# A Fourier mixer and feed-forward kernel: unrolled, with 502-token tiles and a transposed output product

## The reference

```python
X = np.fft.rfft(x, axis=1)                       # along the 3008 tokens
Yr = Xr @ w_r - Xi @ w_i + b_r                   # 256 x 256 weights
Yi = Xr @ w_i + Xi @ w_r + b_i
Y = sign(Y) * maximum(abs(Y) - 0.01, 0)          # of each part
y = np.fft.irfft(Y, n=3008, axis=1)
h = y @ w_in                                     # 256 -> 2048
g = np.maximum(h, 0) + alpha * np.minimum(h, 0)  # alpha: one per hidden unit
out = g @ w_out                                  # 2048 -> 256
```

## Time and profile before

| | |
|---|---|
| median of 3 runs | 1544.65 us (1544.44 to 1545.94) |
| profiled execution, span from first to last instruction | 1542.4 us |
| TensorE matmuls | busy 1452.6 us (94%), 10262 |
| VectorE | 1009.4 us (65%), 2117 |
| ScalarE | 770.3 us (50%), 1901 |
| GpSimd | 232.6 us (15%), 193 |
| DMA | 83.47 MB in 64545 packets, mean 54 GB/s |
| granted TensorE clock, mean | 0.976 |

### The profile page before, as it was taken

The page is one execution under the profiler, slowest core; times in us unless marked ns, Lnnn a source line. Parts: engine busy times, 40 slices in busy tenths (PEclk is TensorE's granted clock), DMA queues, the critical chain, the costliest instruction groups (busy, mean ns, idle before and its releaser), DMA issues.

```text
span 1542.4 us, 33926 instructions
## 1 busy us (share of the span) xinstructions
PE 1452.6 (94%) x10262; PEld 1421.0 (92%) x10262; DVE 1009.4 (65%) x2117; ACT 770.3 (50%) x1901; POOL 232.6 (15%) x193
## 2 busy tenths in 40 slices
PE   2368979999999999999999999999999999999998
PEld 1157879999999999999999999999999999999998
DVE  2247767777677677777677777677767655565654
ACT  1134445555555555555555555555554554555443
POOL 0034431111111111111111111111101010000000
PEclk9997779999999999999999999999999999999999
DMA  2345541111111111111111011111010000000000
GB/s 81 106 143 160 169 130 52 62 48 58 56 50 42 49 61 61 61 48 59 56 50 35 27 41 41 41 41 41 30 41 30 32 21 27 25 20 20 20 10 21
DMA packets 64545, 83.47 MB, mean 54 GB/s; under 512 B 6912, under 2 KB 48256, under 8 KB 64512
## 3 DMA queue, kind: packets, MB, share of 16 engines
q1 hardware_dynamic: 62384, 79.49, 16.5%
q10 hardware_dynamic: 2128, 3.58, 0.7%
...
## 4 chain that ended last, share of the span: by engine, by line
PE 85%; issue 0%; ACT 0%; ACTq 0%
PE out_ps L337 35%; PE h_ps L337 35%; PE work_ps L337 9%; PE work_ps L423 2%; PE work_ps L375 1%; PE work_ps L425 1%; PE work_ps L377 1%; ACT ffw_raw L597 0%; ACTq L83 0%
## 5 line engine op out<-in xcount | busy, mean ns | idle before, releaser
L521 ACT ACTIVATE negpart<-h_ps 128x376 f32<-128x376 f32 x512 | 248.1, 485 | 547.2 <-PE h_ps L337 543.8
L655 DVE SCALAR_TENSOR_TENSOR g_raw<-negpart,keep,h_ps 128x376 f32<-128x376 f32 x512 | 308.7, 603 | 324.2 <-ACT negpart L521 309.3
L337 PE MATMUL out_ps<-wout_hi,g_hi 128*128 128x256 f32 (+1 forms) x1536 | 431.2, 281 | 0.8
L337 PE MATMUL out_ps<-wout_lo,g_hi 128*128 128x256 f32 (+1 forms) x1536 | 431.8, 281 | 0.0
L337 PE MATMUL out_ps<-wout_hi,g_lo 128*128 128x256 f32 (+1 forms) x1536 | 430.4, 280 | 0.0
L337 PE MATMUL h_ps<-y_hi,win_hi 128*128 (+1 forms) x1024 | 351.1, 343 | 2.8 <-DVE y_lo L742 2.8
L337 PE MATMUL h_ps<-y_hi,win_lo 128*128 (+1 forms) x1024 | 343.0, 335 | 0.0
L337 PE MATMUL h_ps<-y_lo,win_hi 128*128 (+1 forms) x1024 | 342.6, 335 | 0.0
L625 DVE TENSOR_TENSOR g_lo<-g_raw,g_hi 128x376 fp32r<-128x376 f32 x512 | 320.2, 625 | 0.1
L337 PEld LDWEIGHTS out_ps<-wout_hi,g_hi 128*128 128x128 f32 (+1 forms) x1536 | 286.0, 186 | 3.1 <-issue 3.1
L337 PEld LDWEIGHTS out_ps<-wout_hi,g_lo 128*128 128x128 f32 (+1 forms) x1536 | 287.0, 187 | 0.0
...
## 6 DMA issues: line engine op xcount, KB each, us to landing
pair_raw<-fwd_scratch SPq DMA_DIRECT2D x32, 384.0 KB, 3.3
inv_scratch<-inv_sb SPq DMA_DIRECT2D x32, 384.0 KB, 2.6
staging<-inv_scratch SPq DMA_DIRECT2D x32, 384.0 KB, 3.6
...
```

The source lines that it names most:

```text
L337: mm = pe.matmul(ps, lhs, rhs, start=(first and m == 0), stop=(last and m == len(terms) - 1), **kw)
L521: act.activation(negpart[:, m % 2, :], h_ps[:, m % 2, 0:TOK], ACT.Relu, scale=-1.0).then_inc(done["negpart"], 1)
L655: dve.scalar_tensor_tensor(g_raw[:, m % 2, :], negpart[:, m % 2, :], keep[:, m:m + 1], h_ps[:, m % 2, 0:TOK], ALU.mult, ALU.add).then_inc( ...
```

## The change

The program is unrolled: no loops, every wait is on a constant, and a count per semaphore stands in place of the helper `wait`. The work is cut anew:

- The feed-forward has 24 tiles, six to a batch, of 502, 502 and 500 tokens. Tokens stand in the order of b first (y is 16 values of b by 94 of a), a tile is a run of that order and may begin and end inside a b.
- `output` takes `w_out` as the stationary operand and `g` as the moving one: 2 halves of the channels x 3 matmuls of 502 columns. `out_ps` has channels on its partitions. VectorE turns it back in blocks of 32 x 32 with `transpose` (`turn`), two or three instructions for each half, into `turned`; ScalarE copies nothing. SP stores it in 12 transfers to a tile, each at most 32 rows with 10 to 12 pieces of 128 B (32 channels).
- `output` follows two steps behind `hidden` (`LAG = 2`), `g_hi` and `g_lo` have three places in place of four.
- Before the feed-forward stands a prologue for batch 0 alone: 16 halves of x, then 24 pairs in a pipeline (in step k TensorE does `forward2(k + 1)`, `inverse2(k - 2)`, `mixing(k)`), with the feed-forward weights split between them, then six units of the inverse. For that time `h_ps` and `out_ps` serve as second banks.
- Behind it the work for the next batch is spread over the six tiles of the current one by `s_unit`, `p_unit` and `i_unit`: x halves one to a step in 16 steps in a row from m = 1 of the first tile, pairs at 9/4 steps apart, inverse units every second step. `x_raw` has three places of one half; in the prologue x's rest is made on VectorE, later on GpSimd. The negated third of `spec_lo` goes from VectorE to GpSimd (`negate`).

The diff, cut to what this text speaks of; the other stages' operations keep their form.

```diff
-TOK = NA * BT
-CHUNK = 32 * BT
-CHUNKS = [min(CHUNK, TOK - c * CHUNK) for c in range(3)]
-OUT_LAG = 3
...
-            phases(pe, body, "SPVIFO")
...
+HALF = 16 * NA
+TILE_AT = ((0, 502), (502, 502), (1004, 500))
+TILES = 6 * BATCH
+TILE_B0 = (0, 5, 10)
+TILE_RUNS = (
+    ((0, 0, 5, 0, 3), (470, 5, 1, 0, 1)),
+    ((0, 5, 1, 1, 2), (62, 6, 4, 0, 3), (438, 10, 1, 0, 2)),
+    ((0, 10, 1, 2, 1), (30, 11, 5, 0, 3)),
+)
+TILE_STORES = (
+    ((0, 0, 6), (1, 0, 5), (2, 0, 5)),
+    ((0, 6, 5), (1, 5, 6), (2, 5, 5)),
+    ((0, 11, 5), (1, 11, 5), (2, 10, 6)),
+)
+TILE_BPAIRS = ((0, 1, 2), (3, 4, 5), (6, 7))
+TILE_UNITS = (6, 12, 16)
+BPAIR_LAST = (0, 0, 1, 1, 1, 2, 2, 2)
+S_UNITS = BATCH * NB // 2
+S_HEAD = NB // 2
+P_UNITS = BATCH * PAIRS
+I_HEAD = 6
+LAG = 2
+PERIOD = 6 * STEPS
+CHUNKS = 8
...
+def s_unit(f, m):
+    at = f % 6 * STEPS + m - 1
+    return S_HEAD * (f // 6 + 1) + at if f < TILES - 6 and 0 <= at < S_HEAD else None
...
+def p_unit(f, m, after):
+    at = f % 6 * STEPS + m - after - 22
+    for j in range(PAIRS):
+        if f < TILES - 6 and at == 9 * j // 4:
+            return PAIRS * (f // 6 + 1) + j
+    return None
...
+def i_unit(f, m):
+    units = [2 * v + h for v in next_bpairs(f) for h in range(DH)]
+    at = m - 4
+    return units[at // 2] if at >= 0 and at % 2 == 0 and at // 2 < len(units) else None
...
+            def load_x(s):
+                if s >= S_UNITS:
+                    return
+                if s >= 3:
+                    sp.wait_ge(x_lo_done, s - 2)
+                g, b = divmod(2 * s, NB)
+                sp.dma_start(x_raw[:, s % 3, :].rearrange("a (b d) -> a b d", b=2),
+                             x_v[:, g, b:b + 2, :]).then_inc(x_loaded[s % 3], 16)
...
+            def store_out(f, n):
+                g, q, (k, b, count) = f // 6, n % 4, TILE_STORES[f % 3][n // 4]
+                sp.wait_ge(turned_done, 2 * f + 2)
+                at, rows, low = b - TILE_B0[f % 3], min(32, NA - 32 * k), f % 6 // 3 * 16 + b
+                sp.dma_start(out_v[g, q, 32 * k:32 * k + rows, low:low + count, :, :].rearrange("a b h e -> a (b h) e"),
+                             turned[32 * q:32 * q + rows, f % 2, k, at:at + count, :, :].rearrange("p b h e -> p (b h) e")
+                             ).then_inc(out_stored[f % 2], 16)
...
+            for s in range(S_HEAD):
+                store_fwd(s)
+                load_x(s + 3)
+                if s in (4, 6):
+                    c = s // 2 - 2
+                    sp.dma_start(mixw_raw[:, c, :, :], (w_r, w_i)[c].rearrange("(h p) e -> p h e", h=DH)
+                                 ).then_inc(mixw_loaded, 16)
+                if s in (8, 10):
+                    load_table(s // 2 - 4)
...
+            for p in range(6):
+                load_pair(p)
+            for c, v in enumerate((b_r, b_i)):
+                sp.dma_start(bias[64 * c:64 * c + 64, :],
+                             v.rearrange("(o e) -> o e", o=1).to_broadcast([64, DIM])).then_inc(bias_loaded, 16)
+            load_ffw(0)
+            load_ffw(1)
...
+            def forward1(s):
+                pe.wait_ge(x_lo_done, s + 1)
+                if s == S_HEAD:
+                    pe.wait_ge(y_lo_done, I_HEAD)
+                elif s > S_HEAD:
+                    pe.wait_ge(fwd_copied, s)
+                    if s % S_HEAD == 0:
+                        pe.wait_ge(inv_copied, PAIRS * (s // S_HEAD))
+                elif s >= 2:
+                    pe.wait_ge(fwd_copied, s - 1)
+                hi, lo = x_hi[:, s % 2, :], x_lo[:, s % 2, :]
+                product(s_bank(s), [(dft_hi[:, :], hi), (dft_hi[:, :], lo), (dft_lo[:, :], hi)]).then_inc(fwd_mm, 1)
...
+            def hidden(f, m):
+                q = f * STEPS + m
+                at, size = TILE_AT[f % 3]
                 if m == 0:
+                    pe.wait_ge(y_lo_done, f // 3 * 16 + TILE_UNITS[f % 3])
+                if f == 0 and m % 2 == 0:
+                    pe.wait_ge(w_lo_done, m // 2 + 1)
+                if q < 2:
+                    pe.wait_ge(spec_lo_done, PAIRS)
+                else:
+                    pe.wait_ge(g_done, q - 1)
                 cols = slice(m % 2 * P, (m % 2 + 1) * P)
                 terms = []
+                for h in range(DH):
                     hi, lo = win_hi[:, m // 2, h, cols], win_lo[:, m // 2, h, cols]
+                    yh, yl = y_hi[:, h, at:at + size], y_lo[:, h, at:at + size]
                     terms += [(hi, yh), (hi, yl), (lo, yh)]
+                product(h_ps[:, q % 2, 0:size], terms).then_inc(h_mm, 1)
...
             def output(f, m):
+                q = f * STEPS + m
+                size = TILE_AT[f % 3][1]
+                pe.wait_ge(g_lo_done, q + 1)
+                if q == 0:
+                    pe.wait_ge(biased_done, PAIRS)
+                gh, gl = g_hi[:, q % 3, 0:size], g_lo[:, q % 3, 0:size]
+                for h in range(DH):
+                    if m == 0 and f >= 1:
+                        pe.wait_ge(turned_done, 2 * f - 1 + h)
+                    d = slice(h * P, (h + 1) * P)
+                    hi, lo = wout_hi[:, m // 2, m % 2, d], wout_lo[:, m // 2, m % 2, d]
+                    mm = product(out_ps[:, h, 0:size], [(hi, gh), (hi, gl), (lo, gh)], first=m == 0, last=m == STEPS - 1)
+                    if h == 0 and m == STEPS - 1:
+                        mm.then_inc(out_half, 1)
+                mm.then_inc(out_mm, 1)
...
+            pe.wait_ge(const_split, 1)
+            for s in range(S_HEAD):
+                forward1(s)
+            for k in range(-1, PAIRS + 2):
+                if k + 1 < PAIRS:
+                    forward2(k + 1)
+                if k >= 2:
+                    inverse2(k - 2)
+                if 0 <= k < PAIRS:
+                    mixing(k)
+            pe.wait_ge(const_split, 2)
+            for u in range(I_HEAD):
+                inverse1(u)
+            for f in range(TILES):
+                for m in range(STEPS):
+                    hidden(f, m)
+                    s = s_unit(f, m)
+                    if s is not None:
+                        forward1(s)
+                    p = p_unit(f, m, 0)
+                    if p is not None:
+                        forward2(p)
+                    p = p_unit(f, m, 3)
+                    if p is not None:
+                        inverse2(p)
+                    p = p_unit(f, m, 1)
+                    if p is not None:
+                        mixing(p)
+                    u = i_unit(f, m)
+                    if u is not None:
+                        inverse1(u)
+                    q = f * STEPS + m - LAG
+                    if q >= 0:
+                        output(*divmod(q, STEPS))
...
+            def bend(f, m):
+                q = f * STEPS + m
+                size = TILE_AT[f % 3][1]
+                dve.wait_ge(negpart_done, q + 1)
+                if q >= 2:
+                    dve.wait_ge(g_hi_done, q - 1)
+                    dve.wait_ge(g_lo_done, q - 1)
+                dve.scalar_tensor_tensor(g_raw[:, q % 2, 0:size], negpart[:, q % 2, 0:size], keep[:, m:m + 1],
+                                         h_ps[:, q % 2, 0:size], ALU.mult, ALU.add).then_inc(g_done, 1)
...
+            def rest_bent(f, m):
+                q = f * STEPS + m
+                size = TILE_AT[f % 3][1]
+                dve.wait_ge(g_hi_done, q + 1)
+                rest(g_lo[:, q % 3, 0:size], g_raw[:, q % 2, 0:size], g_hi[:, q % 3, 0:size]).then_inc(g_lo_done, 1)
...
+            def turn(f, h):
+                if h == 0:
+                    dve.wait_ge(out_half, f + 1)
+                else:
+                    dve.wait_ge(out_mm, STEPS * (f + 1))
+                if f >= 2:
+                    dve.wait_ge(out_stored[f % 2], 16 * 12 * (f // 2))
+                for at, b, count, k, blocks in TILE_RUNS[f % 3]:
+                    ps = bass.AP(out_ps[:, :, :].tensor, h * 512 + at, [[1024, P], [NA, count], [32, blocks], [1, 32]])
+                    b -= TILE_B0[f % 3]
+                    place = turned[:, f % 2, k:k + blocks, b:b + count, h, :].rearrange("p k b e -> p b k e")
+                    op = dve.transpose(place, ps)
+                op.then_inc(turned_done, 1)
...
+            dve.wait_ge(bias_loaded, 32)
+            for k in range(-1, PAIRS + 2):
+                if 0 <= k - 1 < PAIRS:
+                    shrink(k - 1)
+                if k + 1 < PAIRS:
+                    rest_spec(k + 1)
+                if 0 <= k - 1 < PAIRS:
+                    rest_shrunk(k - 1)
+                if 2 <= k + 3 < PAIRS:
+                    rest_pair(k + 3)
...
+            for f in range(TILES):
+                for m in range(STEPS):
+                    bend(f, m)
+                    q = f * STEPS + m
+                    if q >= 1:
+                        rest_bent(*divmod(q - 1, STEPS))
+                    if f >= 1 and m == LAG - 1:
+                        turn(f - 1, 0)
+                        turn(f - 1, 1)
```

(29 more changed lines are left out.)

1072 lines of the change are left out of this document (489 added, 583 removed).

## The result

The changed kernel takes 1566.71 us (median of 4 runs, 1565.6 to 1567.61) beside 1545.05 for the kernel before (4 runs, 1544.44 to 1545.94): a ratio of 1.0143, 95% interval 1.0129 to 1.0158. It is 1.4% slower; 1555 was forecast, 0.7% slower. The profiled execution has a span of 1565.4 us.

The account below looks back on a forecast made before the run. Bound: a 230 us prologue that waits, then 1307 us of back-to-back matmuls. Forecast: prologue 200 + matmuls 1281 + stalls 60 + end 11.5 = 1552.5 us span, plus 2.25 to the median, so 1555; range 1505 to 1592, its own 1548 to 1572.

Parts of the forecast that it names:

- rival 5: The forecast itself: whole kernel slower, 1555 us with bounds of 1548 to 1572; chance 0.36.
- rival 2: Prologue pairs run at VectorE's 2.7 us a step instead of 3.6, so the kernel takes 1524 us; chance 0.17.
- the step by columns: A TensorE matmul costs 0.45 to 0.46 ns a column at every width, so 502 columns take 0.2255 us.
- (a), S zone: Sixteen steps from m = 1 of tiles 0, 6 and 12 wait for x: stalls 37 us, bounds 10 and 65.
- rival 1: The x loads don't bind; only cast and GpSimd's rest stall TensorE, 10 us, so 1528 us; chance 0.25.
- the sum of stalls: TensorE's stalls behind the prologue: x waits 37, output turn 8, shorter lag 12, others 3, together 60 us.
- the loads of the inverse scratch on the same queues 2 more: In tiles 0, 6 and 12, inverse scratch loads sharing the x loads' queues add 2 us to x's arrival.
- (b), the turn: VectorE's transposes of the output hold TensorE's next output product: 0.5 us a switch, 8 us in 23 switches.
- rival 3: Output transposes run at half rate, 1.4 to 1.7 us a half: 30 to 40 us more, 1590; chance 0.12.
- (c), the lag: Output two steps behind hidden instead of three leaves 0.5 us slack for `g_lo`: 12 us of stalls, bounds 0 and 30.
- The end: After the last product, one transposed half, twelve stores issued in 7.3 us and 2.6 to land: 11.5 us.
- another buffer doesn't speed them: Prologue x loads follow one another at 4.29 us each, 45 GB/s, whatever the number of buffers.

Follow-up runs that it names:

- experiment 1: Changed kernel with each x load cut in two: rows 0 to 79 and 80 to 93 took 1495.61 us, rows 0 to 46 and 47 to 93 took 1807.29 us.
- Experiment 7: Changed kernel with the rests of the feed-forward weights in the prologue moved from GpSimd to VectorE: 1565.56 us.
- experiment 4: Changed kernel, x loads cut into 80 and 14 rows, x cast and rest behind the prologue one step earlier (1482.81 us) or rest on VectorE (1482.02 us).
- experiment 2: Changed kernel with the three x loads that fetch ahead moved to steps 12 to 14 of the batch's second tile: 1558.06 us.
- The direct test: Changed kernel with output products three steps behind their hidden products instead of two: 1556.29 us.
- the cut: Each x load split into rows 0 to 79 and 80 to 93: 1490.49 us on the kernel before, 1495.61 us on the changed kernel.
- the best version: Changed kernel with x loads cut into 80 and 14 rows, x rests on VectorE, earlier bias loads, first output product one step later: 1471.01 us.

## Why the prediction was right or wrong

In differences of the spans: prologue -29 us (forecast -30), matmuls behind it -14 (-14), stalls +63 (+48), end +3.4 (+6): +23 against +10.

**The direction and the prologue.** Slower was forecast (rival 5), and the feed-forward starts at 200.7 us, 200 forecast. Errors cancel in it, which is luck. The last x unit comes 7 us later than 71.9, of which 5 are the wait for the table of the inverse DFT (experiment 1), a term that the prediction did not have. VectorE is let go for the first pair at 97 instead of 91. From there to the end of the last pair it takes 89 us and not 94, since the first and last of the 26 steps are short. A pair in between takes 3.58 us (first `shrunk` 101.0, last 183.4), 3.6 forecast, from an estimate of half a GpSimd operation per pair; rival 2 (2.7 us) falls. Experiment 7 shows the hold, but not that the hold alone makes up these 0.9 us.

**TensorE's work.** 0.226 us for 502 columns, 0.2255 forecast, so the step by columns stands. The formula that the prediction weighed against it stands in the Trainium skill, "TensorE: Matmul & The Clock Gate", § Back-to-back issue gap, as the gap of an isolated matmul; for a stream the section gives about 131 ns at 512 columns. The 0.230 us of this case are above both.

**(a), S zone: 37 us forecast, 36.6 measured, by a mechanism that is half right.** The load at 4.3 us is 19 us of it (experiment 1), 11 are the chain of cast and GpSimd's rest (experiment 4), and the remaining 6 stand for the most part in the first steps of these tiles: some 2 are the lower clock at the start of tile 0, which the kernel before had too, the rest was not taken apart. What the clock costs later in these tiles is inside the 19. For tile 0 alone 9 was forecast, and 10.7 to 13.4 came. The prediction had this chain, at 0.2 us a step and only in rival 1; it costs 0.5 to 0.6 in the steps that also carry an inverse unit, where VectorE also has `y` to do.

**The step that failed: the sum of stalls, 60 us where 75 were.** It priced the x loads of tiles 0, 6 and 12 by what they do to the x units. Its term "the loads of the inverse scratch on the same queues 2 more" was the place to ask the converse. Three loads fetched ahead at the end of the run hold two DMA engines for 9 us, and the inverse load that tiles 1 and 7 need is served by all sixteen: 8.6 us (experiment 2), not in the sum at all. The remainder is spread, and not all of it is assigned: inverse units take 0.44 us in place of 0.414, some 3 to 4 us in 122 units, the S zone is up to 2 us more if tile 0 is counted by its own matmuls, and the turn up to 2. The prediction priced all matmuls behind the prologue at 2.4 GHz, and had no term for a clock that falls after these waits; 1.2 us of it are in the 8.6 (step 4 of tile 7 took 8.0 us, that of tile 1 6.8), if the clock is what sets these apart.

**(b), the turn.** 0.3 to 0.5 us a switch in plain tiles and 0.9 in two tiles of each batch, 8 to 10 us in all, 8 forecast; a half takes 0.73 us, so rival 3 falls.

**(c), the lag.** Forecast 12. The direct test gives 4 us in the pair tiles; what it gives in tiles 1 and 7 belongs to the late inverse load. Tiles 2 to 4 take 184.5 us a batch, where their matmuls at the prediction's prices make 180 (an estimate): 13 us in three batches, of which the turn is 5. So 12 for the lag was too much by half or more.

**The end.** 8.8 us, 11.5 forecast: the twelve stores are issued in 5.8 us, not 7.3, and the last has landed 1.8 us later, not 2.6. The device time of a run is 1.8 to 1.9 us over the span of that same run, in all runs on record; the 2.25 of the prediction compared a median with the span of another execution.

**The premise on which all rested.** That "another buffer doesn't speed them", "at 45 GB/s", was read rightly from the casts, but as the speed of a load and not of its cut: the DMA share of 0.29 in that stage already said that most engines did nothing. The Trainium skill, "DMA: Bandwidth & Descriptors", § Why a DMA increments its semaphore by 16 and not by 1, states the rule: a transfer uses the largest number of engines up to sixteen that divides the outermost size on both sides. For 94 rows that is 2, for 47 it is 1, for 80 it is 16. The shares of 0.13, 0.07 and 0.74 in experiment 1 agree. By it the load's pace is a matter of its cut. That a wide transfer behind it is late as well is what tiles 1 and 7 show. Rival 1 (the loads don't bind) falls, though a stall of its kind, 11 us, was there beside them.

**What remains open.** Why the kernel before wins 54 us in its prologue from the cut and the changed kernel 43: both shorten from first cast to last by the pace of the loads (65.2 to 26.3 us and 70.9 to 35.8), and its first `shrunk` comes 52 us earlier against 43. Nor is it known what makes up the 5 us by which the changed kernel is slower when both have the cut. No run takes the remaining pace of 2.4 us a unit apart. In tiles 2 to 4 of each batch the best version still has 4 us of stalls, the turn's included; GpSimd's negation of `spec_lo`, which was on VectorE before, was not tried there.
